# Reordering loads, weight splits and first heads in a one-core kernel of attention and two feed-forward stages

## The reference

```python
# q, k, v: (4, 12, 448, 64); q and k are scaled up by 5.9, moe_w_gate by 22.5
scores = q @ k.T / 8
scores = cap * tanh(scores / cap)              # cap = 30
attn = exp(scores - rowmax); attn /= rowsum + 1e-9
x = (attn @ v), heads side by side             # (1792, 768)
x = (sigmoid(x @ w_gate) * (x @ w_val)) @ w_out        # 768 -> 1536 -> 768
h = x @ w_in;  y = (h * cos(h)) @ w_out2               # 768 -> 2048 -> 768
```

## Time and profile before

| what | value |
|---|---|
| median of 3 runs | 1272.59 us (1270.11 to 1274.39) |
| profiled execution: time | 1272.93 us |
| its span | 1271.1 us |
| TensorE matmul busy | 1244.6 us, 98% |
| VectorE busy | 641.9 us, 50% |
| ScalarE busy | 513.0 us, 40% |
| GpSimd busy | 403.0 us, 32% |
| DMA | 277.61 MB, mean 218 GB/s |
| mean granted TensorE clock | 0.993 |

### The profile page before, as it was taken

The page is one execution under the profiler, slowest core; times in us unless marked ns, Lnnn a source line. Parts: engine busy times, 40 slices in busy tenths (PEclk is TensorE's granted clock), DMA queues, the critical chain, the costliest instruction groups (busy, mean ns, idle before and its releaser), DMA issues.

```text
span 1271.1 us, 17303 instructions
## 1 busy us (share of the span) xinstructions
PE 1244.6 (98%) x6310; PEld 1131.7 (89%) x6310; DVE 641.9 (50%) x1333; ACT 513.0 (40%) x995; POOL 403.0 (32%) x410
## 2 busy tenths in 40 slices
PE   7798999999999999999999999999999999999999
PEld 6567998999999999999999999999999999999998
DVE  6681128876674114886666211687666511104610
ACT  6671125556641114565564111655564211104610
POOL 6569776879754200424000310233100000000000
PEclk8899999999999999999999999999999999999999
DMA  3446996889776766557654766556665456666663
GB/s 105 164 140 225 339 308 215 293 281 320 285 281 236 257 211 207 185 170 236 237 186 151 258 217 208 187 175 205 232 220 181 165 205 210 215 222 212 234 243 112
DMA packets 100452, 277.61 MB, mean 218 GB/s; under 512 B 11152, under 2 KB 19728, under 8 KB 100368
## 3 DMA queue, kind: packets, MB, share of 16 engines
q1 hardware_dynamic: 96912, 271.00, 61.6%
q10 hardware_dynamic: 3456, 5.51, 1.1%
HBM read 217.48 MB, written 58.98 MB: 217 GB/s over the span
## 4 chain that ended last, share of the span: by engine, by line
PE 88%; DVE 4%; POOL 3%; ACT 2%; DMA 2%; issue 1%; SPq 0%; POOLq 0%; ACTq 0%; DVEq 0%
PE acc L577 25%; PE acc L578 25%; PE acc L579 25%; PE t_ps L532 3%; PE acc L567 2%; PE s_ps L499 2%; PE s_ps L500 2%; PE acc L569 2%; DMA qk_in_whole<-qk 2%; POOL qk_in L379 1%; PE t_ps L533 1%; POOL w_lo L379 1%; PE acc L547 1%; DVE rowmax L922 0%; ACT prob L734 0%
## 5 line engine op out<-in xcount | busy, mean ns | idle before, releaser
L577 PE MATMUL acc<-h_hi,w_hi 128*128 128x448 f32 x672 | 251.0, 374 | 0.0
L578 PE MATMUL acc<-h_lo,w_hi 128*128 128x448 f32 x672 | 245.6, 365 | 0.0
L579 PE MATMUL acc<-h_hi,w_lo 128*128 128x448 f32 x672 | 245.4, 365 | 0.0
L577 PE MATMUL acc<-x_hi,w_hi 128*128 128x448 f32 x576 | 211.9, 368 | 4.4 <-POOL w_lo L379 4.4
L578 PE MATMUL acc<-x_lo,w_hi 128*128 128x448 f32 x576 | 211.3, 367 | 0.0
L579 PE MATMUL acc<-x_hi,w_lo 128*128 128x448 f32 x576 | 211.3, 367 | 0.0
L999 DVE SCALAR_TENSOR_TENSOR acc<-scratch,acc 128x448 f32<-128x448 f32 x48 | 30.1, 628 | 237.9 <-PE acc L579 237.9
L577 PE MATMUL acc<-z_hi,w_hi 128*128 128x448 f32 x384 | 140.7, 366 | 0.0
L579 PE MATMUL acc<-z_hi,w_lo 128*128 128x448 f32 x384 | 140.5, 366 | 0.0
L578 PE MATMUL acc<-z_lo,w_hi 128*128 128x448 f32 x384 | 140.5, 366 | 0.0
L579 PEld LDWEIGHTS acc<-h_hi,w_lo 128*128 128x128 f32 x672 | 126.2, 188 | 9.9
(11 more groups left out here) (108 smaller groups left out, 2041.1 us busy)
## 6 DMA issues: line engine op xcount, KB each, us to landing
w_lo<-w_pair SPq DMA_DIRECT2D x156, 384.0 KB, 3.7
w_hi<-w_pair SPq DMA_DIRECT2D x156, 384.0 KB, 3.0
w_lo_whole<-w SPq DMA_DIRECT2D x52, 384.0 KB, 3.8
w_pair<-w_lo SPq DMA_DIRECT2D x52, 384.0 KB, 4.3
w_pair<-w_hi SPq DMA_DIRECT2D x52, 384.0 KB, 4.8
w_lo<-w_pair SPq DMA_DIRECT2D x36, 512.0 KB, 4.3
w_hi<-w_pair SPq DMA_DIRECT2D x36, 512.0 KB, 3.2
qk_in_whole<-qk SPq DMA_DIRECT2D x24, 480.0 KB, 5.9
```

What stands on the lines that cost most here:

```text
L577: e.matmul(out[:, 0:S], w_hi[u % HI][:, wb, :], a_hi[:, kb, :], start=first, stop=False)
L578: e.matmul(out[:, 0:S], w_hi[u % HI][:, wb, :], a_lo[:, kb, :], start=False, stop=False)
L579: return e.matmul(out[:, 0:S], w_lo[u % LO][:, wb, :], a_hi[:, kb, :], start=False, stop=last)
```

## The change

SyncE's list for batch 0's attention is rewritten, and the weight loads are dealt out over it. GpSimd splits three halves of weights in steps 18, 20 and 22 of the attention, and the four heads for batch 1 one at a time behind units 1, 3, 5 and 7. Pair 0 is split by three engines: ScalarE rounds k of both heads, VectorE makes the low k of both and q of head 0, GpSimd makes q of head 1. ScalarE's table is loaded by a tanh on a constant before any data is there. TensorE's second warm-up is five passes and goes ahead of the second group's scores. In batch 0 all normalisations take the form with the zero, also those with n < 0; since the zero of n = -3 lies in acc[3], TensorE waits in unit 11, half 1, for that normalisation.

```diff
-WARM_UP, WARM_KEEP = 10, 4
+WARM_UP, WARM_KEEP = 10, 5
...
-        return 1 if n % NG == 1 else 0
+        return 1 if n == 1 - AHEAD or (n > 0 and n % NG == 1) else 0
...
+            for pr in range(2):
+                for d in range(2):
+                    load_qk(pr, d)
             for d in range(2):
-                load_qk(0, d)
-            load_v_alone(0, 0)
-            for d in range(2):
-                load_qk(1, d)
-            load_v_alone(0, 1)
+                load_v_alone(0, d)
+
             for pr in range(PAIRS):
-                for d in range(2):
-                    load_qk(pr + 2, d)
-                if pr > 0:
-                    load_v_alone(pr, 1)
-                if pr < PAIRS - 1:
-                    load_v_alone(pr + 1, 0)
-                if pr == 1:
-                    for half in halves[:2 * LO]:
-                        load_whole(*half)
+                load_qk(pr + 2, 0)
+                if pr > 1:
+                    load_v_alone(pr - 1, 1)
+                load_qk(pr + 2, 1)
+                if pr > 0:
+                    load_v_alone(pr, 0)
+                for n in ((), (), (0,), (1,), (2, 3), (4, 5))[pr]:
+                    load_whole(*halves[n])
+            load_v_alone(PAIRS - 1, 1)
...
             def qk_high(pr, d):
+                q = queries(pr, d, qk_whole)
                 e.wait_ge(s_qkld[pr % 2][d], 16 * (pr // 2 + 1))
-                rounded(k_hh[pr % 2][d][:, :], keys(pr, d, qk_whole)).then_inc(s_khi[d], 1)
-                e.wait_ge(s_khi[d], pr + d)
                 if pr == 0:
-                    return
-                if pr == 1 and d == 0:
-                    e.wait_ge(s_first_q, 2)
+                    e.wait_ge(s_ident, 1)
+                    e.wait_ge(s_first_low, 1)
+                else:
+                    rounded(k_hh[pr % 2][d][:, :], keys(pr, d, qk_whole)).then_inc(s_khi[d], 1)
+                    e.wait_ge(s_khi[d], pr)
...
-                if stage == 1 and h == 1 and j == 1:
-                    for pr in (first, first + 1):
-                        for d in range(2):
-                            split_qk(pr, d)
+                if stage == 1 and h == 1 and j in (1, 3, 5, 7):
+                    split_qk(first + j // 4, j // 2 % 2)
...
+            early = ((1, 0, 0), (1, 0, 1), (1, 1, 0))
...
+                elif m in (18, 20, 22):
+                    split_w(*early[m // 2 - 9])
...
-                            if b == 0:
+                            if b == 0 and (stage, j, h) not in early:
                                 split_w(stage, j, h)
...
+                        if b == 0 and h == 1 and j == U1 - 1:
+                            e.wait_ge(*normalised(tiles_of(group_of(0, 0))[-1]))
...
-            e.wait_ge(s_pad, PADS)
-            alone(0)
             busy(WARM_KEEP)
-            for m in range(1, STEPS + NG + 2):
+            e.wait_ge(s_pad, PADS)
+            for m in range(STEPS + NG + 2):
                 alone(m)
...
+            e.activation(warm[:, :], half_pi[:, :], ACT.Tanh)
...
+            e.wait_ge(s_qkld[0][1], 16)
+            e.activation(k_hh[0][1][:, :], keys(0, 1, qk_whole), ACT.Copy).then_inc(s_first_k, 1)
...
+            def first_keys(d):
+                e.wait_ge(s_first_k, d + 1)
+                return e.tensor_tensor(keys(0, d), keys(0, d, qk_whole), f32(k_hh[0][d])[:, :], ALU.subtract)
...
-            first_queries(1).then_inc(s_first_q, 1)
+            first_keys(1).then_inc(s_first_low, 1)
...
-                    normalise(group_of(b, n + AHEAD - 1), zeros[idle_output(n)] if b == 0 and n >= 0 else None)
+                    normalise(group_of(b, n + AHEAD - 1), zeros[idle_output(n)] if b == 0 else None)
```

More of the change, by code:

```diff
@@ L140, in build @@
     s_first_kld, s_first_k = sem("k_of_first_head_loaded"), sem("k_hi_of_first_head")
-    s_first_qhi, s_first_q = sem("q_hi_of_first_heads"), sem("q_split_of_first_heads")
+    s_first_qhi, s_first_low = sem("q_hi_of_first_head"), sem("low_parts_of_first_heads")
     s_v0ld, s_vld = [sem(f"v_alone_loaded{d}") for d in range(2)], [sem(f"v_loaded{d}") for d in range(2)]
@@ L381, in qk_high, with qk_low @@
             def qk_high(pr, d):
+                q = queries(pr, d, qk_whole)
                 e.wait_ge(s_qkld[pr % 2][d], 16 * (pr // 2 + 1))
-                rounded(k_hh[pr % 2][d][:, :], keys(pr, d, qk_whole)).then_inc(s_khi[d], 1)
-                e.wait_ge(s_khi[d], pr + d)
                 if pr == 0:
-                    return
-                if pr == 1 and d == 0:
-                    e.wait_ge(s_first_q, 2)
+                    e.wait_ge(s_ident, 1)
[3 more added lines that the diff above has]
+                    e.wait_ge(s_khi[d], pr)
+                rounded(q_hi[D:P, 0:q.shape[1]], q[D:P, :]).then_inc(s_qhi[d], 1)
+                e.wait_ge(s_qhi[d], pr + d)
+            def qk_low(pr, d):
                 q = queries(pr, d, qk_whole)
[L391 to L395, removed]
                 if pr > 0:
-                    q = queries(pr, d, qk_whole)
-                    m = rest(queries(pr, d), q, q_hi[:, 0:q.shape[1]])
-                m.then_inc(s_qk[d], 1)
+                    rest(keys(pr, d), keys(pr, d, qk_whole), k_hh[pr % 2][d][:, :])
+                rest(queries(pr, d), q, q_hi[:, 0:q.shape[1]]).then_inc(s_qk[d], 1)
             def split_qk(pr, d):
@@ L487, in scores @@
                     if pr == 0:
-                        e.wait_ge(s_first_q, part + 1)
+                        e.wait_ge(s_first_low, part + 1)
                 for n, t in enumerate(GROUPS[part]):
@@ L707, in _ @@
             alone(-1)
+            busy(WARM_KEEP)
             e.wait_ge(s_pad, PADS)
-            alone(0)
-            busy(WARM_KEEP)
-            for m in range(1, STEPS + NG + 2):
+            for m in range(STEPS + NG + 2):
                 alone(m)
@@ L896, in _ @@
             e.wait_ge(s_pad, PADS - 1)
[L898 to L908, removed]
+            def first_keys(d):
+                e.wait_ge(s_first_k, d + 1)
+                return e.tensor_tensor(keys(0, d), keys(0, d, qk_whole), f32(k_hh[0][d])[:, :], ALU.subtract)
+            first_keys(0)
+            q = queries(0, 0, qk_whole)
+            e.wait_ge(s_qkld[0][0], 16)
+            e.tensor_scalar(q_hi[D:P, 0:S], q[D:P, :], 1.0, 1.0, ALU.mult, ALU.mult).then_inc(s_first_qhi, 1)
+            e.wait_ge(s_first_qhi, 1)
+            e.tensor_tensor(queries(0, 0), q, f32(q_hi)[:, 0:S], ALU.subtract).then_inc(s_first_low, 1)
             e.wait_ge(s_capd, 1)
@@ L914, in _ @@
             e.memset(f32(qk_in[0][0])[:, 2 * S:QK], 0.0).then_inc(s_pad, 1)
-            e.wait_ge(s_first_q, 1)
-            first_queries(1).then_inc(s_first_q, 1)
+            first_keys(1).then_inc(s_first_low, 1)
             def row_max(g):
```

## The result

The changed kernel takes 1251.5 us (median of 4 runs, 1250.63 to 1251.78), against 1272.7 for the kernel before in the same comparison: a ratio of 0.9834, 95% interval 0.9816 to 0.9852, so 21.2 us less. Forecast were 1252.2 us and 20.4 less.

A forecast was written before the change was run, and what follows sets the result against it. TensorE was taken to bound the kernel, with gains only where it idles or runs at half clock before 122 us. 9.4 + 1.4 + 6.1 + 2.7 + 1.0 = 20.6, less 0.2, gave 1252.2 us, range 1248.5 to 1260.

The forecast's parts named there:

- The order of the loads: Batch 0's attention: SyncE's new list shortens the 20.35 us pair by 8.9 and the 12.14 us pair by 0.5, together 9.4 us.
- The last stretch: Last pair of batch 0's attention: TensorE's 1.40 us of idle goes too, gain 1.4 us, between 0.3 and 1.4.
- the role of the burst: DMA queue in attention: six weight loads issued together ahead of a q/k load made its head usable only 8.35 us later.
- The weight splits: Start of the first product: the 4.38 us wait and 1.7 us lost at half clock go, together 6.1 us.
- GpSimd's pace: First product: with a head on every fourth half, GpSimd needs 3.6 us a half against TensorE's 3.65.
- The first heads: Start of attention: splitting pair 0 on three engines gains 2.7 us, between 0.8 and 3.5.
- the exclusion of the two subtractions: First heads: VectorE's and GpSimd's subtractions block each other, so head 1's matmuls start at 9.2 us instead of 8.5.
- the warm-up passes hold the clock: Start of attention: ten passes, moved ahead, shrink 2.77 us of matmul to some 1.4.
- The zero form: Batch 0's normalisations with n < 0: the zero form removes TensorE's 0.97 us wait at 204.13, between 0 and 1.0.
- GpSimd still waits up to 1.6 us a pair: Rival, attention: GpSimd or the landing bounds a pair, 12.5 us each, time 1257.6 us; chance 0.13.
- no wait for weights came back: Rival, units 2 to 6: spread heads leave GpSimd behind, costing 3 to 6 us, time 1255 to 1258; chance 0.07.
- a clock of 1.00 after 10 us: Sign to look for on TensorE: clock 1.00 after 10 us, beside pair periods of 11.4 to 11.7 us.

The follow-up runs named there:

- a1: The changed kernel with the old list of loads (old order and the burst of six weight halves), the rest new: 1262.76 us.
- b1: The changed kernel with all six weight halves in one burst behind pair 1's loads, new order of q, k and v kept: 1250.81 us.
- b2: The changed kernel with the old order of q, k and v, weight halves dealt out behind pairs 1 to 4 without the burst: 1258.23 us.
- b3: The changed kernel with the three early weight halves, but the four heads in a row behind unit 1: 1251.78 us.
- b4: The changed kernel with spread heads but no early weight halves: 1251.61 us.
- c2: The changed kernel without the five passes of TensorE's second warm-up: 1253.68 us.
- a4: The changed kernel with the tensor-scalar form back for the three groups with n < 0, without TensorE's new wait in unit 11: 1251.42 us.
- c3: The changed kernel without the tanh on a constant that loads ScalarE's table at the start: 1251.87 us.
- c4: The changed kernel with the tensor-scalar form for all 42 tiles of batch 0, without TensorE's new wait in unit 11: 1256.36 us.
- d1: The changed kernel with SyncE holding back the loads of pair 1 and v until head 0 has landed: 1251.76 us.
- a2: The changed kernel with GpSimd's old splits: no early weight halves, four heads in a row behind unit 1: 1259.58 us.

## Why the prediction was right, step by step
*The order of the loads, 9.4 us.* The three pairs became shorter by 0.40, 8.95 and 0.72 us (11.51 to 11.11, 20.35 to 11.40, 12.14 to 11.42): 10.1. Taking the neighbour's period for the long pair was right because TensorE bounds both; the neighbour itself had 0.2 us of idle left, which I did not count. The last stretch gave 23.25 - 21.64 = 1.6 against 1.4. Together 11.7 for 9.4 + 1.4 (the first product begins at 82.98, forecast 84.5), and a1, with 10.5 in the same stretch and 11.3 between the medians, confirms the cause. What the prediction had too simple was the role of the burst. It blamed the wrong order and the burst in one breath; b1 and b2 show that the order is the cause (8.1 us) and the burst only makes a late load later (2.4).

*The weight splits, 6.1 less 0.2 us.* From the first matmul of the product to the scores in unit 10 it takes 162.24 - 82.98 = 79.26 us, before 183.39 - 98.26 = 85.13: 5.9 gained. The step was right in size and over-argued in its parts: I used both edits, while b3 and b4 show that one does it. My sum of GpSimd's pace (3.6 us a half against TensorE's 3.65) left out that TensorE starts 8 us after GpSimd becomes free.

*The first heads, 2.7 us.* 3.6 between the two profiles, 2.3 to 3.0 when counted from the landing, 1.4 to 1.9 between the medians with and without. The first matmul of head 1 follows its data by 2.4 us (5.99 to 8.40; forecast 9.2 - 6.6 = 2.6). For the exclusion of the two subtractions the prediction put 0.7 us, and the trace shows 0.3: GpSimd's, begun at 6.70 while VectorE's ran from 6.55 to 7.18, took 1.60 instead of 1.27, VectorE's its usual 0.63. The row of 1.13 us from which the prediction argued is of another form, a rounding with one input, so it was no measure for a subtraction with two. That the sum came within 0.2 us all the same is luck in part: its other terms were 0.2 short. The prediction's assumption that the warm-up passes hold the clock is shown by c2.

*The zero form, 1.0 us.* The stretch from unit 10's scores to the matmul that waited is 0.78 us shorter (20.74 to 19.96), the wait is gone and comes back in a4; in the time it can't be told.

*The sum.* By the marks in the two traces: 3.60 + 10.07 + 1.61 + 5.87 + 0.78 = 21.9 us at 182 us, of which 0.8 was lost again later (below), 21.2 between the spans. Undoing the parts one at a time costs 11.3 + 8.1 + 1.9 + 0 = 21.3 by the medians; each of these is known to a microsecond or more, so that they add up to within 0.1 is luck, and that they add up to within a few microseconds is what is shown. The rivals: GpSimd still waits up to 1.6 us a pair (for VectorE's reciprocals) and does not bound; no wait for weights came back.

The forecast of a clock of 1.00 after 10 us came true in the profile shown, but not in general. In a4, b4, c3, c4 and d1, with the same second warm-up, 3.4 us between 14 and 19 us run at half clock, here a4:
```profile
15.40:18.60 3.20, 2.99 (x12) 2.32 (x11) 2.08 (x7) 3.20 (x9) 3.20 (x4) 0.50 0.18 73
```
It costs nothing: from landing to pair 1 it takes 11.1 us and from there to the first product 65.8, as without it. The matmuls take longer there, but nobody is held up; ScalarE is busy for all of the 3.20 us. The half clock cost time in c2 and a2, where the next step waited for TensorE, and none here.

No version tried is faster than the changed kernel by more than runs differ. a4, b1, b3, b4 and c3, each simpler in one place, are as fast.

## What to carry to other kernels
A queue that issues loads in a written order should wait for its buffers in the order in which they come free; ask of each wait in it what is queued behind, not what it guards. Read the gain of such a fix from the next stage of the same kind that does not stall, and name the engine that bounds it. When two edits attack one wait, try each alone: here each of two did the whole job, and a burst that looked like a culprit cost nothing once the order gave the load behind it slack.

## What the hardware showed that I had not expected
TensorE has two nearly equal paces at a granted clock of 1.00. In the changed kernel's third product of batch 2, 21 matmuls take 4.34 us, 0.2067 us each; in that of batch 0, 4.26 us, 0.2029 each:
```profile
879.79 0.37 PE L579 MATMUL acc<-z_hi,w_lo 128*128 128x448 f32 x1
...
884.13 0.37 PE L579 MATMUL acc<-z_hi,w_lo 128*128 128x448 f32 x1
```
```profile
299.75 0.36 PE L578 MATMUL acc<-z_lo,w_hi 128*128 128x448 f32 x1
...
304.01 0.36 PE L578 MATMUL acc<-z_lo,w_hi 128*128 128x448 f32 x1
```
In the kernel before it is the other way round: 4.34 us from 299.83 to 304.17, and the quick pace in batch 2. The slow pace ends with a first or third product; it comes with one too, or, in the kernel before and in a2, behind the wait inside the first. It costs 1.1 to 1.5 us in a third product (59.3 or 59.6 us instead of 58.2) and 1.4 in the first. Over the 14 profiles batch 0's first product has it in seven, the third in six, with no relation to the edit. Its cause stays open.

What the quick pace gives in batch 0's third product is in part taken back. In the eight profiles that have it there, TensorE waits twice behind it, 0.5 us together, for VectorE's pt_hi (below, the changed kernel); in the six with the slow pace it doesn't, and the stretch to the next batch's third product is 0.7 to 1.1 us shorter.
```profile
317.61 0.55 PE L532 MATMUL t_ps<-ident,prob 128*128 128x128 f32 x3 [0.26 <-DVE pt_hi L963]
318.50 0.55 PE L532 MATMUL t_ps<-ident,prob 128*128 128x128 f32 x3 [0.23 <-DVE pt_hi L963]
```
So the 0.8 us that the changed kernel loses after 182 us nearly comes out: 1.1 gained in batch 0's third product, 0.7 lost behind it, 1.2 lost in batch 2's. With a landing of head 1 anywhere between 6.0 and 7.7 us in the same profiles, this scatter is larger than an edit worth 1 us, which the medians here can't show; a trace, stage by stage, can.
